# Sliding softmax mix and ELU MLP on one core: TensorE's products over halves of 64 rows, two chunks side by side

## Chip, cores and metric

One core of a Trainium2 chip runs the whole kernel. The time is the device time of one launch in microseconds; lower is better. Three runs of the kernel before gave 1204.01, 1204.09 and 1205.1 us.

## What is computed

`x` is 4 x 4096 tokens of 192 numbers, `weight_gen` has 8 heads x 7 taps for each token. Everything is float32.

```python
w = softmax(weight_gen, axis=-1)                    # with 1e-9 in the divisor
mix[b, s] = sum over k in 0..6 of w[b, s, h, k] * x_pad[b, s + k, h]   # 7 taps, 24 columns a head
h = mix @ w_in                                      # 16384 x 192 times 192 x 2048
g = where(h > 0, h, exp(min(h, 0)) - 1)             # ELU
out = g @ w_out                                     # 16384 x 2048 times 2048 x 192
```

## The kernel before

The 16384 tokens are 32 blocks of 512 (N), four tiles of 128 tokens each. The 2048 hidden columns are 16 chunks of 128. Numbers of float32 that TensorE multiplies are split in two parts that it takes at one pass each, `hi` (rounded by ScalarE's copy) and `lo` (the rest, a subtraction); of a product the parts hi hi, lo hi and hi lo are summed.

- **First product** (`first_product`, L859): for one chunk, a PSUM slot of 128 x 512 is filled by five matmuls of 512 columns. Three contract the first 128 of the 192 rows of the mix. Two contract the other 64 rows; the halves of the 128 rows that the array has there hold those 64 rows twice, as `hi` and as `lo`. Four slots go round. PE writes the slot three chunks (LAG) ahead of the chunk whose second product it does.
- **ELU**: ScalarE takes the exponential of the slot (L649) into `em`, subtracts 1 (L655), VectorE writes max(slot, min(em, 0)) into the slot (L808), ScalarE copies it rounded to `g_hi` (L662), VectorE subtracts for `g_lo` (L814).
- **Second product** (`second_product`): for each of four tiles a matmul with `g_hi` as weights against 384 columns of `wout`, which holds hi and lo side by side (L870), and one with `g_lo` against 192 (L874), into one accumulator bank a tile. In chunks 0 and 15 the two alternate tile by tile. At the end of a block ScalarE copies half of each bank to `cross` (L638) and VectorE adds the other half (L790); this runs in chunk 1 of the next block.
- **The mix**: GpSimd multiplies by the taps (L436) and adds them up (L444, L452, L453, L464, L465), VectorE transposes (L784), SyncE's queue writes to DRAM and reads back turned, ScalarE rounds (L632), GpSimd makes the low parts (L470, L473). The softmax of the block after next is shared by VectorE, GpSimd and ScalarE in steps at fixed chunks of the block.

The order on each engine is that of the code; semaphores tie the engines together.

## Time and profile before

| | |
|---|---|
| median of 3 runs | 1204.09 us |
| the profiled execution, its own time | 1204.23 us |
| its span, first to last instruction | 1202.4 us |
| granted TensorE clock | 0.998 of full speed |
| PE busy | 1183.3 us, 98% |
| weight loads (PEld) busy | 1071.6 us, 89% |
| ScalarE busy | 957.5 us, 80% |
| VectorE busy | 767.7 us, 64% |
| GpSimd busy | 779.2 us, 65% |

PE is the row of matmuls, PEld that of the loads of their weights, which overlap. Busy time is the union of what the profile shows as running. A matmul's end is modelled and reaches past the start of the next, so the start to start time of two matmuls tells more than the duration of one.

### The profile page before, as it was taken

To read this page: it belongs to the slowest core of one execution; us is meant where nothing else is said; L and a number is where in the kernel's file an instruction comes from. 1 tells how busy PE (TensorE), PEld (TensorE's weight loads), DVE (VectorE), ACT (ScalarE), POOL (GpSimd) and SP (SyncE) were. 2 spreads that over 40 slices of the span, in tenths; PEclk is the share of its full clock that TensorE was granted. 3 is DMA by queue.
4 is the path that set the end of the run, shared out by engine and by line. 5 is a ranking of instruction groups with operands and counts; after the bars stand their busy time and mean duration, and the time that the engine had idled before them with its cause. 6 is when DMAs were issued, how large, how long until landed. Compare 5 with 4: busy or idle time off the path is not lost.

```text
span 1202.4 us, 19288 instructions
## 1 busy us (share of the span) xinstructions
PE 1183.3 (98%) x6683; PEld 1071.6 (89%) x6683; DVE 767.7 (64%) x1309; ACT 957.5 (80%) x1786; POOL 779.2 (65%) x359
## 2 busy tenths in 40 slices
PE   5999999999999999999999999999999999999998
PEld 4899999999999999999999999999999999999997
DVE  6666666666656666666666566666666665666655
ACT  5888787887887887878878878878788788788786
POOL 7966785556865567765568655678555686555700
PEclk9999999999999999999999999999999999999999
DMA  7122221222111222112221112221122211221000
GB/s 236 34 81 81 65 67 31 80 81 80 52 51 58 80 80 64 66 31 80 81 80 52 51 58 80 80 64 67 31 80 80 81 51 42 67 80 44 27 31 14
DMA packets 51919, 79.37 MB, mean 66 GB/s; under 512 B 5416, under 2 KB 34852, under 8 KB 51872
## 3 DMA queue, kind: packets, MB, share of 16 engines
q1 hardware_dynamic: 51872, 78.90, 21.5%
q14 instruction: 37, 0.30, 0.1%
q8 instruction: 10, 0.16, 0.1%
HBM read 54.50 MB, written 24.38 MB: 66 GB/s over the span
## 4 chain that ended last, share of the span: by engine, by line
PE 96%; POOL 3%; DMA 0%; issue 0%; DVE 0%; SPq 0%; ACT 0%; DVEq 0%; POOLq 0%
PE slot L859 49%; PE acc L870 29%; PE acc L874 17%; POOL prod L436 1%; POOL prod L444 1%; DMA xwin<-in_x_dram 0%; POOL wout L481 0%; POOL prod L452 0%; POOL prod L453 0%; POOL win_lo L481 0%; POOL win_rest_lo L481 0%; POOL first_mixed L464 0%; POOL first_rest L465 0%; DVE outs L790 0%; PE slot L846 0%
## 5 line engine op out<-in xcount | busy, mean ns | idle before, releaser
L808 DVE SCALAR_TENSOR_TENSOR slot<-em,slot 128x512 f32<-128x512 f32 x512 | 356.3, 696 | 411.6 <-ACT em L655 406.2
L870 PE MATMUL acc<-wout,g_hi 128*128 128x384 f32 x2048 | 461.8, 338 | 0.5 <-DVE g_lo L814 0.5
L649 ACT ACTIVATE em<-slot 128x512 f32<-128x512 f32 x512 | 305.2, 596 | 187.9 <-PE slot L859 187.8
L870 PEld LDWEIGHTS acc<-wout,g_hi 128*128 128x128 f32 x2048 | 372.7, 188 | 43.0 <-issue 1.2
L814 DVE TENSOR_TENSOR g_lo<-slot,g_hi 128x512 fp32r<-128x512 f32 x511 | 349.4, 684 | 0.1
L655 ACT ACTIVATE em<-em 128x512 f32<-128x512 f32 x512 | 323.5, 632 | 16.3
L874 PE MATMUL acc<-wout,g_lo 128*128 128x192 f32 x2048 | 326.0, 266 | 0.0
L874 PEld LDWEIGHTS acc<-wout,g_lo 128*128 128x128 f32 x2048 | 311.2, 190 | 2.4
L436 POOL TENSOR_TENSOR prod<-xwin,probs 128x5376 f32<-128x5376 f32 (+1 forms) x33 | 306.6, 9294 | 6.4 <-POOL xt L473 5.2
L662 ACT ACTIVATE g_hi<-slot 128x512 fp32r<-128x512 f32 x511 | 297.1, 582 | 0.1
L859 PE MATMUL slot<-xt,win_hi 128*128 128x512 f32 (+1 forms) x515 | 215.0, 418 | 1.5 <-ACT xt L582 1.5
L859 PE MATMUL slot<-xt,win_rest_hi 128*128 128x512 f32 (+1 forms) x515 | 204.1, 397 | 0.1
L859 PE MATMUL slot<-xt_lo,win_hi 128*128 128x512 f32 (+1 forms) x515 | 202.5, 394 | 0.2 <-DVE xt_lo L759 0.2
L859 PE MATMUL slot<-xt,win_rest_lo 128*128 128x512 f32 (+1 forms) x515 | 200.3, 390 | 0.0
L859 PE MATMUL slot<-xt,win_lo 128*128 128x512 f32 (+1 forms) x515 | 199.9, 389 | 0.0
L444 POOL TENSOR_TENSOR prod<-prod 128x2304 f32<-128x2304 f32 (+1 forms) x32 | 163.4, 5106 | 2.4
L424 POOL TENSOR_TENSOR wsum<-wsum,eps 128x32 f32<-128x32 f32 x30 | 7.6, 253 | 227.4 <-DVE wsum L553 227.4
L859 PEld LDWEIGHTS slot<-xt_lo,win_hi 128*128 128x128 f32 x515 | 96.8, 188 | 22.7 <-DVE xt_lo L759 0.4
L859 PEld LDWEIGHTS slot<-xt,win_rest_lo 128*128 128x128 f32 x515 | 97.3, 189 | 22.0
L859 PEld LDWEIGHTS slot<-xt,win_rest_hi 128*128 128x128 f32 x515 | 97.1, 189 | 20.7 <-DVE xt L765 0.3
L859 PEld LDWEIGHTS slot<-xt,win_hi 128*128 128x128 f32 x515 | 99.1, 193 | 2.2 <-ACT xt L582 2.2
L859 PEld LDWEIGHTS slot<-xt,win_lo 128*128 128x128 f32 x515 | 99.3, 193 | 0.0
(70 smaller groups left out, 535.0 us busy)
## 6 DMA issues: line engine op xcount, KB each, us to landing
xwin<-in_x_dram SPq DMA_DIRECT2D x29, 960.0 KB, 5.1
out_dram<-outs SPq DMA_DIRECT2D x32, 384.0 KB, 2.6
turned_dram<-turned SPq DMA_DIRECT2D x120, 96.0 KB, 2.0
x_main<-turned_dram SPq DMA_DIRECT2D x30, 256.0 KB, 2.9
x_rest<-turned_dram SPq DMA_DIRECT2D x60, 128.0 KB, 3.0
wg<-in_weight_gen_dram SPq DMA_DIRECT2D x32, 112.0 KB, 2.5
xwin<-in_x_dram SPq DMA_DIRECT2D x2, 768.0 KB, 4.4
wout_raw<-in_moe_w_out_dram SPq DMA_DIRECT2D x4, 384.0 KB, 8.9
```

Of the source, the lines that this page charges most:

```text
L424: nc.gpsimd.tensor_tensor(wsum[:], wsum[:], eps[:], ALU.add).then_inc(s_psoft, 1)
L436: done = nc.gpsimd.tensor_tensor(prod_of(first, end), taps_of(q, first, end), weights_of(q, first, end), ALU.mult)
L444: nc.gpsimd.tensor_tensor(prod[:, 0:half, first_tile * d_model:], prod[:, 0:half, first_tile * d_model:], prod[:, half:2 * half, first_til ...
L649: nc.scalar.activation(em[:, i % 2, :], slot[s][:], ACT.Exp).then_inc(s_exp, 1)
L655: nc.scalar.activation(em[:, i % 2, :], em[:, i % 2, :], ACT.Copy, bias=-1.0).then_inc(s_em, 1)
L662: nc.scalar.activation(g_hi[:, f % GBUFS, :], slot[slot_of(b, pos - 1)][:], ACT.Copy).then_inc(s_ghi, 1)
L808: nc.vector.scalar_tensor_tensor(out=slot[s][:], in0=em[:, i % 2, :], scalar=0.0, in1=slot[s][:], op0=ALU.min, op1=ALU.max).then_inc(s_g, 1)
L814: nc.vector.tensor_tensor(g_lo[:, f % GBUFS, :], slot[slot_of(b, pos - 1)][:], g_hi[:, f % GBUFS, :].bitcast(F32), ALU.subtract).then_inc( ...
L859: return pe.matmul(slot[s][:, tokens], w, v, start=(k == 0), stop=(k == PASSES - 1))
L870: pe.matmul(acc[j][:, 0:2 * d_model], g_hi[:, f % GBUFS, chunk(j)], wout[:, f, :], start=(f == 0), stop=False)
L874: return pe.matmul(acc[j][:, d_model:2 * d_model], g_lo[:, f % GBUFS, chunk(j)], wout[:, f, 0:d_model], start=False, stop=(f == CHUNKS - 1))
```

## The change

- The 192 rows are cut in three pieces of 64. The lower half of the array's rows (0 to 63) works for chunk `2m`, the upper half (64 to 127) for chunk `2m+1`. The mix stands twice in `xt`, once in each half. The weights of even chunks lie in partitions 0 to 63, those of odd ones in 64 to 127. A pair of chunks takes 3 parts x 3 pieces x 2 halves, 18 matmuls of 64 rows and 512 columns, into two slots (`half_products`, L873 of the kernel after).
- The second product of a pair (`second_products`, L900) is done in 64-row halves as well: 16 matmuls of 384 columns with `g_hi`, then 16 of 192 with `g_lo`, in steps of four. In a step the lower half's matmul writes tile j's bank and the upper half's that of tile j+2. Each step waits on `s_row` until the step before the last is complete. The last pair of a block alternates hi and lo by step.
- PE fills the slots of pair m+1 ahead of the second product of pair m.
- In pairs 4 to 7 of a block (`low_first`) VectorE writes min(slot, 0) to `em` (L796), ScalarE takes only the exponential for the odd chunk, and VectorE's L801 subtracts 1 and takes the maximum. `cross` is gone: VectorE sums the two halves of a bank by a reduction (L789), between its two ELU steps and its two subtractions of pair 0.
- The softmax is begun three blocks ahead, the turned mix comes back as three pieces by two reads, ScalarE rounds three pieces (L635), GpSimd makes three low parts (L489), and the final sum of the mix is one instruction. The weights are split by ScalarE and VectorE alone, and w_in is loaded by six transfers a part.

```diff
+        def low_first(m):
+            return m >= PAIRS // 2
...
-            return (6, 11) if b.first else (5, 10)
+            return (4, (0, 3)) if b.first else (3, (0, 3)) if not b.has_old and b.pair == 0 else (2, (1, 2))
...
+        def softmaxes(b):
+            if not b.has_previous:
+                return {("max", 0): 2, ("exp", 1): 2, ("sum", 1): 2, ("rec", 3): 2,
+                        ("max", 5): 3, ("exp", 7): 3, ("sum", 7): 3}
+            late = 6 if b.has_old else 7
+            at = {("rec", 0): 2, ("max", 4): 3, ("exp", late): 3, ("sum", late): 3}
+            return {k: n for k, n in at.items() if number(b) + n < BLOCKS}
...
+                for m in range(PAIRS):
+                    one, two = 2 * m, 2 * m + 1
+                    exponential(b, one)
+                    if low_first(m):
+                        exponential_of_low(b, two)
+                        less_one(b, one)
+                        high(b, two)
+                        high(b, one)
                     else:
+                        less_one(b, one)
+                        exponential(b, two)
+                        less_one(b, two)
+                        high(b, one)
+                        high(b, two)
+                    if b.first and m in SPLIT_AT:
+                        hi_half(*SPLIT_AT[m])
+                    if ("exp", m) in softmax:
+                        softmax_exp(ahead(b, softmax["exp", m]))
+                    if b.has_next and m == at + 2:
+                        high_parts(b, range(pieces[0] or PIECES))
+                    if b.has_next and m == at + 3 and pieces[0]:
+                        high_parts(b, range(pieces[0], PIECES))
...
+                for j, t in enumerate(DONE):
+                    dve.wait_ge(s_row, b.count(STEPS, STEPS - TILES + 1 + j - n_before * STEPS))
+                    nc.vector.tensor_reduce(outs[:, parity, t, :],
+                                            acc[t][:, 0:2 * d_model].rearrange("p (k d) -> p d k", k=2), AX.X,
...
+            def below(b, f):
+                dve.wait_ge(s_filled, b.count(CHUNKS, f + 1))
+                nc.vector.tensor_scalar_min(em[:, 1, :], slot[slot_of(f)], 0.0).then_inc(s_low, 1)
+            def elu_of_low(b, f):
+                dve.wait_ge(s_exp, b.count(CHUNKS, f + 1))
+                nc.vector.scalar_tensor_tensor(out=slot[slot_of(f)], in0=em[:, 1, :], scalar=-1.0,
+                                               in1=slot[slot_of(f)], op0=ALU.add, op1=ALU.max).then_inc(s_g, 1)
+            def elu(b, f):
+                dve.wait_ge(s_em, ems(b, f // 2) + f % 2 + 1)
+                nc.vector.scalar_tensor_tensor(out=slot[slot_of(f)], in0=em[:, f % 2, :], scalar=0.0,
+                                               in1=slot[slot_of(f)], op0=ALU.min, op1=ALU.max).then_inc(s_g, 1)
...
+                for m in range(PAIRS):
+                    one, two = 2 * m, 2 * m + 1
+                    softmax_step("rec", m)
+                    if m == turn_at(b)[0] and b.has_next:
+                        turn(b)
+                    if low_first(m):
+                        below(b, two)
+                        elu_of_low(b, two)
+                        elu(b, one)
+                        low(b, two)
+                        low(b, one)
+                    else:
+                        elu(b, one)
+                        elu(b, two)
+                        if m == 0 and b.has_previous:
+                            dve.wait_ge(s_stored[1 - q], b.per_parity(16, 16 * q))
+                            outputs(b, 1, 1 - q)
+                        low(b, one)
+                        low(b, two)
+                    if b.first and m in SPLIT_AT:
+                        low_half(*SPLIT_AT[m])
+                    softmax_step("max", m)
+                    softmax_step("sum", m)
...
-            def one_pass(parity, f, s, k, tokens=slice(0, N)):
-                cols = chunk(f)
-                w, v = ((win_hi[:, cols], xt[:, parity, 0, tokens]), (win_lo[:, cols], xt[:, parity, 0, tokens]),
-                        (win_hi[:, cols], xt_lo[:, parity, tokens]), (win_rest_hi[:, cols], xt[:, parity, 1, tokens]),
-                        (win_rest_lo[:, cols], xt[:, parity, 1, tokens]))[k]
-                return pe.matmul(slot[s][:, tokens], w, v, start=(k == 0), stop=(k == PASSES - 1))
-            def first_product(parity, f, s):
-                for k in range(PASSES):
-                    last = one_pass(parity, f, s, k)
-                last.then_inc(s_filled, 1)
...
+            def half_products(parity, m, passes, tokens=slice(0, N)):
+                cols = chunk(m)
+                for n in passes:
+                    k = n % PIECES
+                    w, v = ((win_hi, xt), (win_lo, xt), (win_hi, xt_lo))[n // PIECES]
+                    for h, rows in enumerate(HALVES):
+                        last = pe.matmul(slot[slot_of(2 * m + h)][:, tokens], w[rows, k, cols],
+                                         v[rows, parity, k, tokens], start=(n == 0), stop=(n == PASSES - 1))
+                        if n == PASSES - 1 and tokens.stop == N:
+                            last.then_inc(s_filled, 1)
+            def second_products(b, m):
+                one, two = 2 * m, 2 * m + 1
+                hi = (g_hi, slice(0, 2 * d_model))
+                lo = (g_lo, slice(d_model, 2 * d_model))
+                highs, lows_ = ((one, hi), (two, hi)), ((one, lo), (two, lo))
+                if m == PAIRS - 1:
+                    steps = [(j, highs + lows_) for j in range(TILES)]
                 else:
-                    pe.wait_ge(s_ghi, b.count(CHUNKS, f + 1))
-                    for j in range(TILES):
-                        hi(j)
-                    pe.wait_ge(s_split, b.count(CHUNKS, f + 1))
-                    for j in range(TILES):
-                        last = lo(j)
-                    last.then_inc(s_used, 1)
+                    steps = [(j, part) for part in (highs, lows_) for j in range(TILES)]
+                pe.wait_ge(s_ghi, b.count(CHUNKS, two + 1))
+                for step, (j, products) in enumerate(steps):
+                    if m == 0 and step < 2:
+                        ge(pe, s_out, b.count(TILES, 2 * step + 2 - TILES))
+                    ge(pe, s_row, b.count(STEPS, 4 * TILES * m + 2 * step - 2))
+                    for n, (f, (g, cols)) in enumerate(products):
+                        if j == 0 and f == one and g is g_lo:
+                            pe.wait_ge(s_split, b.count(CHUNKS, two + 1))
+                        for h, rows in enumerate(HALVES):
+                            t = (j + 2 * h) % TILES
+                            last = pe.matmul(acc[t][:, cols], g[rows, f % GBUFS, chunk(t)],
+                                             wout[rows, f, 0:cols.stop - cols.start],
+                                             start=(f == 0 and g is g_hi and step < 2),
+                                             stop=(f == CHUNKS - 1 and g is g_lo and j >= 2))
+                            if n == len(products) - 1:
+                                last.then_inc(s_row, 1)
...
+                for m in range(PAIRS):
+                    n = m + 1
+                    if n < PAIRS:
+                        if not (b.first and n < 2):
+                            ge(pe, s_split, b.count(CHUNKS, 2 * (n - 1)))
+                            if b.first and n % 2 == 0:
+                                pe.wait_ge(s_wlo, SPLITS.index(("in", n // 2)) + 1)
+                            half_products(q, n, range(PASSES))
                     elif b.has_next:
-                        i = f + LAG - CHUNKS
-                        if i == 0:
-                            if b.has_previous:
-                                pe.wait_ge(s_xtlo, b.count(2))
-                            else:
-                                pe.wait_ge(s_xlo, 2 * XPARTS * X_STEPS)
-                        slot_free(len(steps) + i)
-                        first_product(1 - q, i, i % SLOTS)
-                    if not b.has_previous and f in (p.start for p in WOUT_PARTS):
-                        part = f // (CHUNKS // 4)
-                        if ("out", part) in LO_ORDER:
-                            pe.wait_ge(s_wlo, LO_ORDER.index(("out", part)) + 1)
-                        else:
-                            pe.wait_ge(s_plo, PLO_ORDER.index(("out", part)) + 1)
-                    second_product(b, f)
+                        pe.wait_ge(s_xtlo, b.count(PIECES, PIECES))
+                        pe.wait_ge(s_split, b.count(CHUNKS, CHUNKS - 2))
+                        half_products(1 - q, 0, range(PASSES))
+                    if b.first and m % 2 == 0:
+                        pe.wait_ge(s_wlo, SPLITS.index(("out", m // 2)) + 1)
+                    second_products(b, m)
```

TensorE in the middle of a block. Before, from the last matmul of a first product to the next one (a name is written tile, then `<-` and what is read):

```order
L859 MATMUL slot<-xt,win_rest_hi 128x512
L859 MATMUL slot<-xt,win_rest_lo 128x512
L870 MATMUL acc<-wout,g_hi 128x384 [waits s_ghi]
L870 MATMUL acc<-wout,g_hi 128x384 x3
L874 MATMUL acc<-wout,g_lo 128x192 [waits s_split]
L874 MATMUL acc<-wout,g_lo 128x192 x3
L859 MATMUL slot<-xt,win_hi 128x512 [waits s_split]
```

After, one pair of chunks: the rest of its first products and the first two steps of the second products:

```order
L873 MATMUL slot<-xt,win_hi 128x512 x5
L873 MATMUL slot<-xt,win_lo 128x512 x6
L873 MATMUL slot<-xt_lo,win_hi 128x512 x6
L900 MATMUL acc<-wout,g_hi 128x384 [waits s_row,s_ghi]
L900 MATMUL acc<-wout,g_hi 128x384 x3
L900 MATMUL acc<-wout,g_hi 128x384 [waits s_row]
L900 MATMUL acc<-wout,g_hi 128x384 x3
```

A chunk's 5 + 4 + 4 matmuls have become a pair's 18 + 16 + 16, and a wait on `s_row` stands ahead of each four matmuls of a second product; two more such steps with `g_hi` and four with `g_lo` follow.

VectorE at the start of a block. Before, around the four sums of the block before:

```order
L814 TENSOR_TENSOR g_lo<-slot,g_hi 128x512 [waits s_ghi]
L790 TENSOR_TENSOR outs<-acc,cross 128x192 [waits s_cross,s_stored1]
L790 TENSOR_TENSOR outs<-acc,cross 128x192 [waits s_cross] x3
L808 SCALAR_TENSOR_TENSOR slot<-em,slot 128x512 [waits s_em]
L814 TENSOR_TENSOR g_lo<-slot,g_hi 128x512 [waits s_ghi]
```

After, from the last steps of the softmax ahead of pair 0 to pair 1:

```order
L562 TENSOR_REDUCE wsum<-probs 128x32 [waits s_esoft]
L566 RECIPROCAL wrec<-wsum 128x32 [waits s_psoft]
L807 SCALAR_TENSOR_TENSOR slot<-em,slot 128x512 [waits s_em] x2
L789 TENSOR_REDUCE outs<-acc 128x192 [waits s_row,s_stored0]
L789 TENSOR_REDUCE outs<-acc 128x192 [waits s_row] x3
L813 TENSOR_TENSOR g_lo<-slot,g_hi 128x512 [waits s_ghi] x2
L807 SCALAR_TENSOR_TENSOR slot<-em,slot 128x512 [waits s_em] x2
L813 TENSOR_TENSOR g_lo<-slot,g_hi 128x512 [waits s_ghi] x2
```

The four sums now stand between the ELU steps (L807) and the subtractions (L813) of pair 0, on which PE's `g_lo` steps wait.

## Rows read from the trace of the kernel before

**Rows 1.** The page: busy time by engine, and the chain that ended last.

```profile
PE 1183.3 (98%) x6683; PEld 1071.6 (89%) x6683; DVE 767.7 (64%) x1309; ACT 957.5 (80%) x1786; POOL 779.2 (65%) x359
...
PE slot L859 49%; PE acc L870 29%; PE acc L874 17%; POOL prod L436 1%; POOL prod L444 1%; DMA xwin<-in_x_dram 0%; POOL wout L481 0%; POOL prod L452 0%; POOL prod L453 0%; POOL win_lo L481 0%; POOL win_rest_lo L481 0%; POOL first_mixed L464 0%; POOL first_rest L465 0%; DVE outs L790 0%; PE slot L846 0%
```

**Rows 2.** The waits: who waited for whom, us in total, times, longest.

```profile
DVE slot L808 <- ACT em L655: 406.2, 452, 2.0
...
ACT em L649 <- PE slot L859: 187.8, 377, 1.9
```

**Rows 3.** Timeline, one chunk and a third: start us, us, engine, line, operation, tiles.

```profile
601.54 0.60 ACT L649 ACTIVATE em<-slot 128x512 f32<-128x512 f32 x1 [0.54 <-PE slot L859]
...
602.17 0.63 ACT L655 ACTIVATE em<-em 128x512 f32<-128x512 f32 x1
...
602.46 0.42 PE L859 MATMUL slot<-xt,win_hi 128*128 128x512 f32 x1
...
602.71 0.58 ACT L662 ACTIVATE g_hi<-slot 128x512 fp32r<-128x512 f32 x1
602.72 0.39 PE L859 MATMUL slot<-xt,win_lo 128*128 128x512 f32 x1
...
602.84 0.69 DVE L808 SCALAR_TENSOR_TENSOR slot<-em,slot 128x512 f32<-128x512 f32 x1 [1.00 <-ACT em L655]
602.95 0.39 PE L859 MATMUL slot<-xt_lo,win_hi 128*128 128x512 f32 x1
...
603.41 0.39 PE L859 MATMUL slot<-xt,win_rest_lo 128*128 128x512 f32 x1
...
603.44 0.68 DVE L814 TENSOR_TENSOR g_lo<-slot,g_hi 128x512 fp32r<-128x512 f32 x1
603.64 0.86 PE L870 MATMUL acc<-wout,g_hi 128*128 128x384 f32 x4
603.84 0.60 ACT L649 ACTIVATE em<-slot 128x512 f32<-128x512 f32 x1 [0.55 <-PE slot L859]
...
604.34 0.58 PE L874 MATMUL acc<-wout,g_lo 128*128 128x192 f32 x4
...
604.76 0.42 PE L859 MATMUL slot<-xt,win_hi 128*128 128x512 f32 x1
```

**Rows 4.** Groups by line: busy us, mean ns of one, idle before and releaser.

```profile
L870 PE MATMUL acc<-wout,g_hi 128*128 128x384 f32 x2048 | 461.8, 338 | 0.5 <-DVE g_lo L814 0.5
...
L874 PE MATMUL acc<-wout,g_lo 128*128 128x192 f32 x2048 | 326.0, 266 | 0.0
...
L790 DVE TENSOR_TENSOR outs<-acc,cross 128x192 f32<-128x192 f32 x128 | 37.1, 351 | 13.7 <-ACT cross L638 12.6 <-ACT cross L682 1.1
...
L632 ACT ACTIVATE xt<-x_main 128x512 fp32r<-128x512 f32 x30 | 18.7, 624 | 0.0
...
L549 DVE TENSOR_REDUCE wmax<-wg 128x32 f32<-128x224 f32 x30 | 11.3, 377 | 0.0
```

**Rows 5.** Timeline, the last chunk: a weight load that waited, and those behind it.

```profile
1197.47 0.19 PEld L870 LDWEIGHTS acc<-wout,g_hi 128*128 128x128 f32 x1 [0.18 <-DVE g_lo L836]
1197.48 0.44 PE L870 MATMUL acc<-wout,g_hi 128*128 128x384 f32 x1
...
1197.76 0.25 PE L874 MATMUL acc<-wout,g_lo 128*128 128x192 f32 x1
...
1197.85 0.36 PE L870 MATMUL acc<-wout,g_hi 128*128 128x384 f32 x1
...
1198.04 0.25 PE L874 MATMUL acc<-wout,g_lo 128*128 128x192 f32 x1
```

**Rows 6.** Timeline of the start: w_in's transfers, and the split that waits for them.

```profile
3.06 1.18 SPq L323 DMA_DIRECT2D win_rest_raw<-in_moe_w_in_dram  x2
...
9.50 0.63 ACT L597 ACTIVATE win_hi<-win_raw 128x512 fp32r<-128x512 f32 x1 [5.48 <-DMA win_rest_raw<-in_moe_w_in_dram]
```

517 lines of the change are left out of this document (197 added, 320 removed).

## Prediction

> **What bounds the kernel now.** I read the page first. PE is busy 98% of the span, and the chain that ended last is PE through and through: 49% in the first products and 29% + 17% in the second ones [rows 1]. Next the waits: ScalarE waited 187.8 us in all for PE's slots, and VectorE 406.2 us for ScalarE [rows 2]. The helpers wait for PE and PE for nobody, so only what shortens PE's own stream counts. Last the timeline of one chunk, from start to start: the first product from 602.46 to 603.64 is 1.18 us, the four matmuls of 384 columns up to 604.34 are 0.70, the four of 192 up to 604.76 are 0.42, together 2.30 us, and 4.60 for two chunks [rows 3]. Per matmul that is 0.23 for 512 columns (0.26 for the first of the five), 0.174 for 384 and 0.105 for 192. The granted clock is 0.998 of full speed, that is the 2.4 GHz level, where a column a tick would make 0.213, 0.160 and 0.080 (the step from 384 to 512 columns, 0.056, is near the 0.053 of that). What is left for the swap of weights is 0.014 to 0.017, and more, 0.025, at 192 columns.
>
> **TensorE's stream.** I call a matmul of the lower half and the one of the upper half behind it a couple. If the two halves of a couple run side by side, it costs what one matmul of its width costs now. The first products of a pair are then 9 couples, 0.26 + 8 x 0.23 = 2.10 us, where two chunks took 2 x 1.18 = 2.36. The second products are 8 couples at 0.174 = 1.39 and 8 at 0.105 = 0.84, as long as now. The pair takes 4.33 us in place of 4.60. That is the upper end of this case: 256 pairs x 0.27 = 69 us less. The lower end lets the swap of one half's weights hide under the other half's columns: 9 x 0.213 + 8 x 0.160 + 8 x 0.09 = 3.92 us (0.09 is what a matmul of 192 columns takes between two of 384, from 1197.76 to 1197.85 [rows 5]), 0.68 x 256 = 174 us less. No row shows a 64-row matmul. The nearest rows are today's, and each half still swaps between two of its own matmuls, so I stay near the upper end, a third of the way down: 4.19 us, 0.41 x 256 = **-105 us**.
>
> A pair has 50 weight loads where it had 26. The Trainium skill ("TensorE: Matmul & The Clock Gate", LDWEIGHTS) says that a load's time goes by its columns and not by its rows, 128 columns at 1.2 GHz, so a 64-row load would cost as much as a full one. The trace agrees as far as it goes, since 0.105 us is what the narrowest matmuls need. The Trainium skill's "TensorEngine Tiling (Array Packing)" (Key Properties) says that different tiles can load and multiply in parallel; no run here shows that yet. By the second rule the sum stands; with loads that cost this much one behind the other it would be near the first rival's.
>
> **The row waits.** Each step of four matmuls waits until the step before the last is complete. For 384 columns: the last matmul of that step shows 0.338 us [rows 4], and a semaphore takes some 0.04 (PE's last matmul ends at 603.41 + 0.39 = 603.80, ScalarE starts at 603.84 [rows 3]). From its start that is 0.38, and the step that waits is due 0.174 + 2 x 0.174 = 0.52 after it. No loss. For 192 columns: 0.266 + 0.04 = 0.31 against 0.105 + 0.21 = 0.315; it arrives in time, but the weights cannot be loaded ahead. What that costs is in the last chunk: the load at 1197.47 waited for its semaphore, and the next matmul started 0.28 after its own matmul's start, against 1198.04 - 1197.85 = 0.19 for the same two undisturbed [rows 5], so 0.09. Two chains of steps interleave, so at most about 0.1 a pair, at least nothing. I take 0.05 x 256 = **+13 us**.
>
> **The helpers, pair by pair.** Let e be the end of a pair's last first-product matmul. In pairs 0 to 3, with the start to start times of [rows 3]: ScalarE's exponential at e + 0.04, minus one at 0.67, the second exponential at 1.21, its minus one at 1.84, done at 2.47; VectorE at 2.51, done at 3.20; ScalarE's `g_hi` at 3.24, done at 3.82, seen at 3.86, and with a weight load that waited, 3.95. PE is there 4.19 - 0.39 + 0.23 = 4.03 after e. The cover is 0.08 us, which is thin. Under 4.11 us a pair these four pairs would be bound by ScalarE and VectorE. In pairs 4 to 7 the chain is exponential to 0.73, VectorE's minimum beside it (not in this trace; the nearest row is its 0.69 on the same slot), exponential to 1.40, VectorE 1.41 to 2.7 for both chunks, `g_hi` of the second to be rounded done at 3.3, 3.4 with the hop; 0.6 us of cover. One minus-one of 0.63 is gone from ScalarE there; three roundings of 0.62 a block in place of two [rows 4] lie in that cover. GpSimd's and the softmax's work was moved by blocks, not by the microsecond, and GpSimd is at 65% [rows 1]; I cost it at nothing. If that cover is gone, PE waits for the turned mix at the end of a block.
>
> **The start of a block.** Here is the one wait that I see for sure. VectorE has its second ELU step of pair 0 at e + 2.51 and can go on at 3.11 (a step of 0.60). Then come four reductions of 384 numbers. None is in the trace: one of 224 numbers takes 0.377 [rows 4], one more number about 1 ns (512 numbers 0.684, 192 numbers 0.351), so 0.54 each, started every 0.46. They end at 5.03. PE's first step of pair 0 needs two of them and is about in time; its second is due at 4.03 + 0.35 = 4.38, needs all four, and starts at 5.03 + 0.04 + 0.09 = 5.16: 0.78 lost. Behind the reductions the two subtractions end at 4.95 + 0.60 + 0.68 = 6.23, and PE, at 5.16 + 3 x 0.35 = 6.19, needs them at 6.36 with hop and load: 0.17 more. Together 0.95 x 31 blocks = **+29 us**. The bounds are 0 (the adds of today, 0.351 each, cost PE nothing, but there PE had three chunks in hand) and 1.5 us a block if the strided reduction runs at 0.68.
>
> **Start and end.** w_in comes in six transfers a part where three were issued, 1.18 us for two of them, and ScalarE's first split waits 5.48 us for the data [rows 6]: +2 us. In the first block ScalarE and VectorE also split the weights that GpSimd did: +1. At the end the last pair has no first products ahead of it: its `g_hi` comes 3.95 us after e, PE has only 2.2 us of pair 6: +2. Sum **+5 us**, 2 to 10.
>
> **Sum.** From the profiled execution's own 1204.2 us (span 1202.4; the median is 0.1 less): 1204.2 - 105 + 13 + 29 + 5 = **1146 us**.
>
> **The rivals.**
> *Loads or issue queue up* (slower). If the two halves' loads, or the instructions, go one behind the other at the 0.105 us that a load and a matmul need at least today [rows 3], each couple of the second product costs 0.21 and the pair 2.10 + 16 x 0.21 = 5.46 us; +220, with PE so slow that the waits vanish: 1429 us. It decides from 0.145 us a couple. For it: no row shows two in less. Against it: that 0.105 is measured with all 128 rows in one load, and the two halves need not share it. The Trainium skill ("TensorE: Matmul & The Clock Gate", Back-to-back issue gap) has 81 ns for a load and a 128-column matmul in a stream; by an estimate from that page, 0.162 a couple of 192 columns, the time would be some 1250 us. No run here shows it.
> *Row waits cost a blocked load each* (slower). Eight a pair at 0.085 are 0.68 us: 1133 + 174 = 1307 us. It decides from three in eight. Against it: the sum above leaves 0.14 us of room at 384 columns.
> *The helpers bind.* The chain of pairs 0 to 3 is 0.25 us longer than reckoned: (0.25 - 0.08) x 128 = 22 and a little more at block starts: 1175 us, still faster.
> *The halves do not run side by side.* Then the change does not do what it says: 18 x 0.23 + 16 x 0.174 + 16 x 0.105 = 8.6 us a pair, 2230 us.
>
> **How the numbers follow.** Forecast 0.50 (own range 1080 to 1170), helpers bind 0.20 (1165 to 1200), loads or issue 0.13, row waits 0.11, not side by side 0.03, and 0.03 that gain and waits cancel. Faster 0.70, within 0.2% (which is about what a measurement here can tell) 0.03, slower 0.27. The range 1080 to 1240 holds the first two, the cancelling and the mild part of the next two, about 0.8.
>
> **What the profile after would show.** Right: the matmuls of a couple start within some 10 ns of each other, couples of 512 columns 0.21 to 0.23 apart, of 192 columns 0.08 to 0.11; PE waits once a block for VectorE's reductions, near 1 us; ScalarE waits for PE less than 187.8 us in all. Wrong: starts of a couple 0.1 us or more apart (loads or issue), or as far apart as a whole matmul (not side by side), gaps ahead of every fourth matmul (row waits), or PE waiting for `g_hi` in pairs 0 to 3 (helpers). A reduction of over 0.6 us, or a clock that PE's new gaps let fall from 1.0, would make the number wrong though the mechanism is right.

## The result, and the profile after

| | before | after |
|---|---|---|
| median | 1204.05 us (4 runs) | 1246.21 us (4 runs, 1245.63 to 1246.66) |
| span of the profiled execution | 1202.4 us | 1244.9 us |
| granted TensorE clock, mean | 0.998 | 0.99 |

The ratio is 1.0348, with a 95% interval of 1.033 to 1.0366. The changed kernel is 3.5% slower, where the forecast was 1146 us with a range up to 1240.

The page of the kernel after; the first row answers to the first of [rows 1], the second and third are the chain that ended last:

```profile
PE 1200.8 (96%) x12848; PEld 1026.3 (82%) x12848; DVE 922.7 (74%) x1431; ACT 903.0 (73%) x1549; POOL 802.3 (64%) x355
...
PE 81%; DVE 7%; ACT 5%; issue 5%; POOL 2%; DMA 0%; DVEq 0%; SPq 0%; POOLq 0%
PE acc L900 44%; PE slot L873 37%; DVE outs L789 5%; ACT em L642 3%; ACT em L652 2%; POOL prod L453 1%; DMA xwin<-in_x_dram 0%; DVE slot L807 0%; DVE win_lo L760 0%; POOL xt_lo L489 0%; DVE wout L760 0%; POOL prod L470 0%; POOL prod L469 0%; DVE acc L730 0%; PE slot L861 0%
```

PE is still the bound, but no longer alone: the chain goes through VectorE, ScalarE and GpSimd for 14% of the span, the largest part of it, 5%, in L789, the four reductions of a block. The waits of the kernel after answer to [rows 2]:

```profile
ACT em L642 <- PE slot L873: 217.9, 249, 3.1
DVE slot L807 <- ACT em L652: 173.0, 186, 3.7
...
ACT em L647 <- DVE em L796: 31.5, 126, 10.4
...
PE acc L900 <- issue: 11.3, 2, 9.2
...
PE acc L900 <- DVE outs L789: 8.5, 31, 0.3
```

ScalarE waits for PE more than before (217.9 us where it was 187.8), not less as I had written. Two rows are new: PE waits 31 times for the reductions, and one of ScalarE's waits for VectorE's minimum lasted 10.4 us.

The groups that answer to [rows 4]:

```profile
L900 PE MATMUL acc<-wout,g_hi 64*128 64x384 f32 x4096 | 434.5, 341 | 25.3 <-issue 11.3 <-DVE outs L789 8.5 <-ACT g_hi L658 5.6
...
L900 PE MATMUL acc<-wout,g_lo 64*128 64x192 f32 x4096 | 334.1, 288 | 0.1
...
L789 DVE TENSOR_REDUCE outs<-acc 128x192 f32<-128x384 f32 x128 | 62.3, 548 | 2.6 <-PE acc L900 2.6
```

**One pair of chunks.** TensorE's timeline of the kernel after, the last pair of a block, whose second products alternate hi and lo by step:

```profile
600.38 0.88 PE L873 MATMUL slot<-xt,win_hi 64*128 64x512 f32 x6
601.10 0.86 PE L873 MATMUL slot<-xt,win_lo 64*128 64x512 f32 x6
601.79 0.85 PE L873 MATMUL slot<-xt_lo,win_hi 64*128 64x512 f32 x6
602.48 0.51 PE L900 MATMUL acc<-wout,g_hi 64*128 64x384 f32 x4
602.82 0.36 PE L900 MATMUL acc<-wout,g_lo 64*128 64x192 f32 x4
...
604.74 0.65 PE L873 MATMUL slot<-xt,win_hi 64*128 64x512 f32 x4
```

Six matmuls of 512 columns take 0.69 us (601.10 to 601.79), so a couple takes 0.23. The halves do run side by side. The pair is 604.74 - 600.38 = 4.36 us, beside the 4.33 of my upper end. The same timeline where all `g_hi` steps stand ahead of the `g_lo` ones, as in pairs 0 to 6:

```profile
612.17 1.58 PE L900 MATMUL acc<-wout,g_hi 64*128 64x384 f32 x16
...
613.58 1.27 PE L900 MATMUL acc<-wout,g_lo 64*128 64x192 f32 x16
...
614.69 0.88 PE L873 MATMUL slot<-xt,win_hi 64*128 64x512 f32 x6
```

The 16 matmuls with `g_hi` take 1.41 us (I had reckoned 1.39), but the 16 with `g_lo` take 1.11 where I had 0.84. Such a pair takes 4.61 us, the 4.60 of two chunks before: all that the halves gain is lost again in the `g_lo` steps. Narrow windows on these 16 matmuls give the start of each step; here are the second and the fourth:

```profile
613.83 0.36 PE L900 MATMUL acc<-wout,g_lo 64*128 64x192 f32 x2
...
614.39 0.36 PE L900 MATMUL acc<-wout,g_lo 64*128 64x192 f32 x2
```

The eight couples of `g_lo` start at 613.58 and 613.68 (first step), 613.83 and 614.02 (second), 614.13 and 614.25 (third), 614.39 and 614.58 (fourth), and the next first product at 614.69. Where nothing waits they stand 0.10 to 0.12 apart. The second and the fourth step start 0.15 and 0.14 behind the couple ahead of them, and in both the second couple comes 0.19 behind the first. Each of these two steps loses some 0.12 us; the first and the third lose nothing.

**One block.** Read in this way from start to start of the first products, the eight pairs of each block from the third on take 4.61, 4.35, 5.33, and then five times 4.61; from 563.02 to 600.38 that is 37.36 us, where a block before took 36.75 (1102.40 / 30). The 5.33 is the stretch with pair 0's second products:

```profile
605.72 1.95 DVE L789 TENSOR_REDUCE outs<-acc 128x192 f32<-128x384 f32 x4
...
606.87 0.61 PE L900 MATMUL acc<-wout,g_hi 64*128 64x384 f32 x4
...
607.59 1.28 DVE L813 TENSOR_TENSOR g_lo<-slot,g_hi 128x512 fp32r<-128x512 f32 x2
607.60 9.71 POOL L453 TENSOR_TENSOR prod<-xwin,probs 128x5376 f32<-128x5376 f32 x1 [0.16 <-POOL probs L448]
...
607.80 1.32 PE L900 MATMUL acc<-wout,g_hi 64*128 64x384 f32 x12 [0.32 <-DVE outs L789]
```

The reductions end at 607.67 (605.72 + 1.95), PE's second step starts at 607.80, and the stretch is 0.72 us longer than the others. That wait is the one that was forecast (0.95).

**The first 100 us.** Busy time and granted clock by stretch, before and after:

```profile
0.00:50.00 50.00, 34.42 (x176) 29.62 (x177) 32.43 (x57) 36.22 (x68) 42.90 (x31) 0.97 0.52 162
50.00:100.00 50.00, 50.00 (x287) 45.37 (x286) 32.77 (x60) 39.41 (x79) 38.27 (x15) 1.00 0.16 49
```

```profile
0.00:50.00 50.00, 31.06 (x284) 27.05 (x284) 41.48 (x48) 25.96 (x43) 41.08 (x24) 0.93 0.50 152
50.00:100.00 50.00, 38.07 (x374) 33.10 (x372) 35.05 (x49) 29.20 (x51) 29.45 (x12) 0.86 0.23 62
```

The columns are the stretch, its length, busy us (and instructions) of PE, PEld, VectorE, ScalarE and GpSimd, the granted clock, the DMA share and GB/s. PE is busy 12 us less in the second stretch than before, and its clock is 0.86 there. Four rows of the timeline say why:

```profile
44.45 9.71 POOL L453 TENSOR_TENSOR prod<-xwin,probs 128x5376 f32<-128x5376 f32 x1 [0.27 <-POOL probs L448]
...
44.80 10.17 DVE L760 TENSOR_TENSOR win_lo<-win_raw,win_hi 128x768 fp32r<-128x768 f32 x1
...
59.22 2.93 PE L900 MATMUL acc<-wout,g_hi 64*128 64x384 f32 x16 [9.20 <-issue]
59.88 0.96 DVE L760 TENSOR_TENSOR wout<-wout_raw,wout 128x768 fp32r<-128x768 f32 x1
```

A subtraction for the weights' low parts takes VectorE 0.96 us at 59.88 and 10.17 us at 44.80. It starts just behind a product of GpSimd's and ends at 54.97, 0.81 us after that product's end at 54.16. VectorE's ELU steps are queued behind it, ScalarE waits 10.4 us for the minimum, and PE stands for 9.20 us. After that its 16 `g_hi` matmuls need 2.70 us from start to start (59.22 to 61.92), 1.9 times the 1.41 of later; the granted clock from 59.2 to 61.9 is 0.50, which is the 1.2 GHz level and not the 2.4.

**The sum.** PE runs ahead with its first products, so a block is counted here up to the start of its last first product (that of pair 7, or of chunk 15 before). "Start" is the start of the very first one, and "rest" is what follows the last one:

| | start | blocks 0, 1 | 30 blocks | rest | span |
|---|---|---|---|---|---|
| before | 13.54 | 76.76 | 1102.40 | 9.7 | 1202.4 |
| after | 14.86 | 95.13 | 1120.99 | 13.92 | 1244.9 |
| difference | +1.3 | +18.4 | +18.6 | +4.2 | +42.5 |

And for a later block: eight pairs at 4.36 would be 34.88, 1.87 less than before. The `g_lo` steps of seven pairs add 1.76 and the reductions 0.72. So a gain of 1.87 stands against a loss of 2.48: +0.61, which is 18.3 over thirty blocks. In the rest, the last pair's first `g_hi` step starts at 1236.74, and PE had stood 0.98 us for it; its second products then take 4.2 us, at a granted clock of 0.65, where the same pair takes 2.26 in the steady blocks.

### The profile page after: what moved, and what is told of

Read it like the earlier page. It is cut to its first block, busy times and chain, and to the rows that moved or that the text cites. A ratio compares the mean times of both kernels' runs of the same rounds, so it can differ in the third digit from the quotient of the medians.

```text
span 1244.9 us, 33016 instructions
## 1 busy us (share of the span) xinstructions
PE 1200.8 (96%) x12848; PEld 1026.3 (82%) x12848; DVE 922.7 (74%) x1431; ACT 903.0 (73%) x1549; POOL 802.3 (64%) x355
## 4 chain that ended last, share of the span: by engine, by line
PE 81%; DVE 7%; ACT 5%; issue 5%; POOL 2%; DMA 0%; DVEq 0%; SPq 0%; POOLq 0%
PE acc L900 44%; PE slot L873 37%; DVE outs L789 5%; ACT em L642 3%; ACT em L652 2%; POOL prod L453 1%; DMA xwin<-in_x_dram 0%; DVE slot L807 0%; DVE win_lo L760 0%; POOL xt_lo L489 0%; DVE wout L760 0%; POOL prod L470 0%; POOL prod L469 0%; DVE acc L730 0%; PE slot L861 0%
## 5 line engine op out<-in xcount | busy, mean ns | idle before, releaser
L900 PE MATMUL acc<-wout,g_hi 64*128 64x384 f32 x4096 | 434.5, 341 | 25.3 <-issue 11.3
L900 PEld LDWEIGHTS acc<-wout,g_hi 64*128 64x128 f32 x4096 | 337.4, 186 | 86.3 <-issue 23.6
L807 DVE SCALAR_TENSOR_TENSOR slot<-em,slot 128x512 f32<-128x512 f32 x384 | 266.4, 695 | 173.4 <-ACT em L652 173.0
L642 ACT ACTIVATE em<-slot 128x512 f32<-128x512 f32 x384 | 227.5, 592 | 217.9 <-PE slot L873 217.9
L489 POOL TENSOR_TENSOR xt_lo<-x_raw,xt 128x512 fp32r<-128x512 f32 x93 | 118.5, 1290 | 371.2 <-ACT xt L635 371.2
L813 DVE TENSOR_TENSOR g_lo<-slot,g_hi 128x512 fp32r<-128x512 f32 x512 | 346.5, 689 | 5.5
L900 PE MATMUL acc<-wout,g_lo 64*128 64x192 f32 x4096 | 334.1, 288 | 0.1
L900 PEld LDWEIGHTS acc<-wout,g_lo 64*128 64x128 f32 x4096 | 298.9, 188 | 34.6 <-PE acc L900 6.8
L873 PE MATMUL slot<-xt,win_hi 64*128 64x512 f32 (+1 forms) x1548 | 226.6, 398 | 2.0 <-ACT xt L592 1.3
L873 PE MATMUL slot<-xt,win_lo 64*128 64x512 f32 (+1 forms) x1548 | 221.0, 390 | 0.0
L873 PE MATMUL slot<-xt_lo,win_hi 64*128 64x512 f32 (+1 forms) x1548 | 218.0, 387 | 0.0
L873 PEld LDWEIGHTS slot<-xt,win_lo 64*128 64x128 f32 x1548 | 145.7, 186 | 33.9
L873 PEld LDWEIGHTS slot<-xt_lo,win_hi 64*128 64x128 f32 x1548 | 145.6, 185 | 32.7
L801 DVE SCALAR_TENSOR_TENSOR slot<-em,slot 128x512 f32<-128x512 f32 x128 | 89.1, 696 | 89.4 <-ACT em L647 89.4
L873 PEld LDWEIGHTS slot<-xt,win_hi 64*128 64x128 f32 x1548 | 127.8, 189 | 14.1 <-issue 1.0
L796 DVE TENSOR_SCALAR em<-slot 128x512 f32<-128x512 f32 x128 | 88.5, 691 | 37.4 <-PE slot L873 36.0
L789 DVE TENSOR_REDUCE outs<-acc 128x192 f32<-128x384 f32 x128 | 62.3, 548 | 2.6 <-PE acc L900 2.6
```

Of the source, the lines that this page charges most:

```text
L489: nc.gpsimd.tensor_tensor(by_tile(xt_lo[:, parity, k, :]), by_quad(x_raw[:, k, :]), by_tile(xt[:, parity, k, :].bitcast(F32)), ALU.subtrac ...
L642: nc.scalar.activation(em[:, f % 2, :], slot[slot_of(f)], ACT.Exp).then_inc(s_exp, 1)
L789: nc.vector.tensor_reduce(outs[:, parity, t, :], acc[t][:, 0:2 * d_model].rearrange("p (k d) -> p d k", k=2), AX.X, ALU.add).then_inc(s_ou ...
L801: nc.vector.scalar_tensor_tensor(out=slot[slot_of(f)], in0=em[:, 1, :], scalar=-1.0, in1=slot[slot_of(f)], op0=ALU.add, op1=ALU.max).then_ ...
L807: nc.vector.scalar_tensor_tensor(out=slot[slot_of(f)], in0=em[:, f % 2, :], scalar=0.0, in1=slot[slot_of(f)], op0=ALU.min, op1=ALU.max).th ...
L813: nc.vector.tensor_tensor(g_lo[:, f % GBUFS, :], slot[slot_of(f)], g_hi[:, f % GBUFS, :].bitcast(F32), ALU.subtract).then_inc(s_split, 1)
```

## The experiments

My theory after the result had three parts: the row waits cost about 0.25 us a pair, the reductions 0.72 us a block, and VectorE's blocked splits, with the fallen clock, most of the 18 us of the first two blocks. The rivals were that the `g_lo` steps are slow by their loads or by their banks, that the start is slow for other reasons, and that the losses are not independent.

### Row waits or banks

In pairs 0 to 6 each half of the array keeps two banks of its own, so the two halves never write the same bank and the waits can go without a race. (The banks then hold other sums.) The control has the same banks and keeps the waits.

```diff
-                    ge(pe, s_row, b.count(STEPS, 4 * TILES * m + 2 * step - 2))
+                    if m == PAIRS - 1:
+                        ge(pe, s_row, b.count(STEPS, 4 * TILES * m + 2 * step - 2))
...
-                            t = (j + 2 * h) % TILES
+                            t = (j + 2 * h) % TILES if m == PAIRS - 1 else j % 2 + 2 * h
```

> A measuring kernel: in pairs 0 to 6 the lower half of the array adds into banks 0 and 1 alone and the upper half into banks 2 and 3 alone, so the two never meet in a bank and the waits on s_row ahead of the steps are left out there. The sums land in the wrong tiles, so the output is not the reference's; the instructions, their widths and their number stay. Theory A (the row waits make the narrow steps late): the 16 matmuls of 192 columns take 0.84 us in place of 1.11, a pair 4.33 to 4.36 in place of 4.61, and 7 pairs x 32 blocks x 0.26 = 58 us go: about 1188 us. Theory B (0.07 us is the least for a load and a matmul of 64 rows, whatever waits): the pair stays at 4.61 and the time at 1246 us.

> The same banks as the kernel without the row waits, but with the waits left in: the sums land in the wrong tiles here too. It tells the banks' own effect from that of the waits. Both theories: 4.61 us a pair, 1246 us. If it is faster than that, the choice of banks and not the wait sets the pace.

Measured, one run each: 1194.82 us without the waits, 1242.34 with them, 47.5 us apart; the banks alone make 3.9 us (1246.21 to 1242.34). The timeline of the first one:

```profile
600.78 1.57 PE L901 MATMUL acc<-wout,g_hi 64*128 64x384 f32 x16
602.19 1.03 PE L901 MATMUL acc<-wout,g_lo 64*128 64x192 f32 x16
603.06 0.88 PE L873 MATMUL slot<-xt,win_hi 64*128 64x512 f32 x6
```

The `g_lo` steps take 0.87 us, near the 0.84 of my sum, and the pair 4.37. The waits are the cause and the banks are not. One reason that it is 47.5 and not 7 x 32 x 0.25 = 56 is pair 0, where PE waits for the reductions as well: it comes down only from 5.33 to 5.15, so the two losses of that pair overlap.

### Keep row waits, but give them room

Matmuls with `g_hi` and `g_lo` alternate in pairs 1 to 7, as they did in pair 7 alone. Four of `g_hi` and four of `g_lo` make one step now, so a pair has four row waits in place of eight, and each looks back over a whole step of eight matmuls.

```diff
+    MIXED = 1
...
-                if m == PAIRS - 1:
+                if m >= MIXED:
                     steps = [(j, highs + lows_) for j in range(TILES)]
```

> Undoes one part of the change for pairs 1 to 6: their second product alternates g_hi and g_lo tile by tile, as only the last pair of a block does in the changed kernel (there a pair takes 4.36 us against 4.61). Both theories: pairs 4 to 7 take 4.36 us. In pairs 1 to 3 g_lo is needed earlier than it is there: it comes 4.67 us after the first product's end, which makes a pair 4.48 us. A block is then 37.36 - 3 x 0.25 - 3 x 0.13 = 36.2 us, 31 blocks 36 us less: about 1210 us. Rival: the wait for g_lo eats the gain in pairs 1 to 3 in full, then 0.75 a block is left and 1223 us.

Measured: 1202.39 us, ratio to the kernel before 0.9982 (0.9972 to 0.9991). TensorE's timeline:

```profile
600.89 0.51 PE L905 MATMUL acc<-wout,g_hi 64*128 64x384 f32 x4
601.24 0.37 PE L905 MATMUL acc<-wout,g_lo 64*128 64x192 f32 x4
601.45 0.53 PE L905 MATMUL acc<-wout,g_hi 64*128 64x384 f32 x4
```

Four hi and four lo matmuls together take 0.56 us (600.89 to 601.45) and the pairs 4.36, but for pair 0's 5.33 and one a block at 4.51; I had expected three at 4.48, so it came out 8 us better. 43.8 us come back from the order of the matmuls, with the banks and the sums as they were. The edit changes two things together, the number of waits and the room of each, and no run separates them.

### Is the rest of the stream bound by loads?

`g_lo` meets 96 columns of `wout` in place of 192, once in the kernel without row waits and once in the kernel before. Half of the lo products is left out.

> A measuring kernel on top of the one with own banks and no row waits: the g_lo matmuls of 64 rows have 96 columns in place of 192 (the output is not the reference's: sums in the wrong tiles and half of the g_lo term left out). There 16 of 192 columns took 0.87 us, 0.109 a couple. If the loads of weights set that pace, each half loading its own, it stays at 0.107 a couple and the kernel at 1195 us. If the columns did, it falls to 0.06 a couple, a pair to 3.98 us, and 256 x 0.38 = 97 us go, as far as the helpers allow (they need 4.11 us in pairs 0 to 3): about 1110 to 1130 us.

> The kernel before with 96 columns in place of 192 in its g_lo matmuls of 128 rows (half of the g_lo term is left out, so the output is not the reference's). If a load of 128 rows takes the 0.105 us that these matmuls show, nothing changes: 1204 us. If the columns or a fixed cost beside them set it, four of them take 0.26 in place of 0.42 us and 512 x 0.16 = 82 us go: 1122 us. It tells whether g_lo's matmuls were bound by their loads before the change, and so what the 64-row halves could win or lose there.

Measured, one run each: 1197.93 us beside the 1194.82 with 192 columns, and 1211.17 us beside 1204. Half the columns give next to nothing back. In the changed kernel's variant the thirty later blocks take 1069.7 us in place of 1072.4, and the longer time comes from the first two, where the granted clock from 50 to 100 us is 0.76 and not 0.90; in the variant of the kernel before the same blocks take 1109.2 in place of 1102.4. The timelines, first of the changed kernel's variant, then of the variant of the kernel before:

```profile
601.79 0.99 PE L901 MATMUL acc<-wout,g_lo 64*128 64x96 f32 x16
602.61 0.93 PE L873 MATMUL slot<-xt,win_hi 64*128 64x512 f32 x6
```

```profile
600.70 0.54 PE L874 MATMUL acc<-wout,g_lo 128*128 128x96 f32 x4
601.08 0.46 PE L859 MATMUL slot<-xt,win_hi 128*128 128x512 f32 x1
601.38 0.40 PE L859 MATMUL slot<-xt,win_lo 128*128 128x512 f32 x1
```

Eight couples in 0.82 us are 0.103 a couple; four full matmuls in 0.38 are 0.095 each. The two differ only because the first of a row of narrow ones is followed after 0.05: from the second on they start 0.11 apart in both, and in the kernel without row waits the couples of 192 columns do too. So the columns do not set the pace of the narrow matmuls. A couple has two loads of 64 rows, which start together in the trace (both at 604.65 in the changed kernel), and takes the time of one load and matmul of 128 rows: the loads of the two halves also go side by side. That it is the load that sets the 0.11, and not another cost that every matmul has, is likely but not shown. What is saved there is given back in the next first product (0.30 in place of 0.26, and 0.77, from 602.61 to 603.38, in place of 0.72 for six).

### The reductions at the start of a block

The first of the four reductions goes between VectorE's two ELU steps of pair 0, where VectorE waits for ScalarE.

```diff
                         elu(b, one)
+                        if m == 0 and b.has_previous:
+                            dve.wait_ge(s_stored[1 - q], b.per_parity(16, 16 * q))
+                            outputs(b, 1, 1 - q, (0,))
                         elu(b, two)
                         if m == 0 and b.has_previous:
-                            outputs(b, 1, 1 - q)
+                            outputs(b, 1, 1 - q, (1, 2, 3))
```

> VectorE's four reductions at a block's start: the first one now stands between its two ELU steps of pair 0, where it waits for ScalarE anyway, and three stand behind. Theory (PE's 0.72 us a block is the wait for the fourth reduction and for the subtractions behind it): both come 0.46 us sooner, the wait shrinks to about 0.3, 31 x 0.4 = 12 us go: 1234 us. Rival: the first bank isn't complete in time, the second ELU step is late for it, g_hi too, and nothing is won or a little lost: 1246 to 1252 us.

Measured: 1231.10 us, ratio 1.0224 (1.0207 to 1.0241), 15.1 us under the changed kernel. VectorE's timeline:

```profile
596.47 0.70 DVE L809 SCALAR_TENSOR_TENSOR slot<-em,slot 128x512 f32<-128x512 f32 x1 [1.51 <-ACT em L652]
...
597.08 0.55 DVE L791 TENSOR_REDUCE outs<-acc 128x192 f32<-128x384 f32 x1
597.63 0.70 DVE L809 SCALAR_TENSOR_TENSOR slot<-em,slot 128x512 f32<-128x512 f32 x1
598.23 1.48 DVE L791 TENSOR_REDUCE outs<-acc 128x192 f32<-128x384 f32 x3
```

The last three reductions take 1.48 us in place of 1.95 for four. The stretch is 4.87 in place of 5.33 and the block 36.84 in place of 37.36: 0.5 x 31 = 15.

### VectorE's blocked splits

GpSimd's products for the mix are issued in quarters, so that VectorE waits for one of some 2.7 us and not for 9.7. First for all blocks:

```diff
-                products(q, 0, TILES)
+                for t in range(TILES):
+                    products(q, t, t + 1, last=t == TILES - 1)
```

> GpSimd's large multiplication (9.7 us) is issued as four of a tile each, in every block. Theory: VectorE's splits of the weights in block 0 (L760, both inputs in SBUF) stand still while a GpSimd instruction that reads SBUF runs, and one of them lasts 10.17 us for that reason, beside 3.44 and 4.01; with quarters none lasts over 3.5 us, PE's gap of 9.2 us before pair 4 of block 0 shrinks by 7 us, and the time is about 1238 us. Rival (the splits are slow by themselves, or VectorE waits out all four parts one after the other): the split still lasts 10 us and the time stays at 1246 us or rises by what four smaller instructions cost GpSimd, which has the room.

Measured: 1237.33 us (1234.16 to 1249.42), ratio 1.0263 (1.0239 to 1.0287). One split still lasts 5.83 us, longer than the 3.5 that I had named as the most: it stands beside the pair sum of 5.16 us, which this edit leaves whole. Then for blocks 1 and 2 alone, with the pair sum of block 1 in quarters too:

> The changed kernel, with GpSimd's products for blocks 1 and 2 issued in quarters (and the pair sum of block 1 too), all later blocks as they were. Theory (VectorE's weight splits read SBUF twice and stand still as long as one GpSimd instruction runs beside them, PE then waits and its clock falls): as in the kernel with quarters everywhere, no split of the weights takes over about 6 us, blocks 0 and 1 come to some 89 us in place of 95, and without the extra instructions of the later blocks the time is 1236 to 1240 us. Rival (the gain of the kernel with quarters everywhere came from later blocks): blocks 2 to 31 stay at 37.3 us and the time stays at 1246 us.

Measured: 1240.57 us (1233.73 to 1252.3), ratio 1.0281 (1.0251 to 1.0311) without the longest. VectorE's timeline of the second one, three of its five splits:

```profile
26.10 1.43 DVE L770 TENSOR_TENSOR wout<-wout_raw,wout 128x768 fp32r<-128x768 f32 x1
...
40.95 1.17 DVE L770 TENSOR_TENSOR win_lo<-win_raw,win_hi 128x768 fp32r<-128x768 f32 x1
48.85 1.47 DVE L770 TENSOR_TENSOR wout<-wout_raw,wout 128x768 fp32r<-128x768 f32 x1
```

The splits that took 3.44, 4.01, 2.11, 10.17 and 0.96 us take 1.43, 2.20, 1.24, 1.17 and 1.47, and the first two blocks 82.5 us in place of 95.1. So the splits are blocked as long as one instruction of GpSimd's lasts, and that is shown. The 12.6 us from there would make 1233.6, and the lowest times of the two kernels are 1234.16 and 1233.73. The medians are higher because both kernels scatter, so that a median near the one expected proves little. Their profiled executions are the longest of each, and have two and three pairs that take 8.7 to 9.0 us in place of 4.35 (with the pair behind them, 5 to 6.7 us lost each time). The profile puts PE's pause down to VectorE's `g_lo`, but the one that PE's code asks for there was done long before: 327.87 for a pause from 330.6 to 335.05. The loop instructions of PE (L109) tell more. In the window 329 to 336 of the second kernel:

```profile
L109 PEldq COMPARE_BRANCH  x1: 5077/5077/5077, 329.8 to 329.8; - x1
```

The branch that closes PE's loop over the blocks lasts 5.08 us there and 0.21 as a rule. All five pauses are such branches, of 4.73 to 5.08 us, and the changed kernel's 14 take 0.24 at most. So PE stands at the turn of its own loop; no other engine is shown that holds it. What the branch waits for is open. The row of DMA queue 8, which carries instructions, has 47 packets in this execution and 38 in the other, and 20 in the changed kernel's:

```profile
q8 instruction: 47, 0.77, 0.3%
```

That would fit a branch that waits for the instructions behind it, but no run shows it. The quarters alone don't bring it about: the kernel with all three repairs below has them too, has 19 packets, and its four times lie within 1.6 us.

### VectorE's minimum of PSUM

Pairs 4 to 7 do their ELU steps as pairs 0 to 3 do; the minimum (L796) and L801 are gone and ScalarE subtracts the 1.

```diff
         def low_first(m):
-            return m >= PAIRS // 2
+            return False
```

> Undoes VectorE's minimum alone: all pairs go as pairs 0 to 3, with two exponentials from the slot and two times minus one on ScalarE. Theory (at 4.61 us a pair ScalarE has 0.45 us to spare on its way to g_hi): only pair 5, with two roundings of the mix, runs over, by about 0.5 us: 30 x 0.5 = 15 us more, 1261 us. Rival (the minimum is needed in no pair, since the helpers keep up at this pace): 1246 us. Second rival (ScalarE binds all over): over 1290 us.

Measured: 1244.11 us, ratio 1.0332 (1.0315 to 1.0349). The pairs that took 4.61 stay at 4.60. The theory that the minimum carries these pairs fell and its rival held: at 4.6 us a pair ScalarE has the time for the step that VectorE took over.

### All three repairs, and the minimum again

> The changed kernel with hi and lo steps alternating in pairs 1 to 7, and VectorE's first reduction between its two ELU steps of pair 0. Theory (row waits and the start of a block are two separate losses): they add, 44 us from the one and 15 from the other, so 1202.4 - 15 = 1187 us, block period near 35.5 us. Rival (with pairs at 4.36 us VectorE has less room, so that the first ELU steps of pair 0, now later, hold PE up): the second gain shrinks to under 5 us, 1198 us or more.

> As the kernel with alternating steps and the moved reduction, and GpSimd's products for blocks 1 and 2 in quarters. Theory: the three losses add, 1187 - 7 = about 1180 us, 2% faster than the kernel before. Rival (at the start of the launch another wait takes the place of the one removed): no less than 1185 us.

> As the kernel with all three edits, without VectorE's minimum of PSUM: pairs 4 to 7 do their ELU steps as pairs 0 to 3 do. At 4.61 us a pair the minimum made no difference. Theory: at 4.36 us the chain of ScalarE and VectorE in pairs 1 to 3, the same as it would now be in 4 to 7, keeps up (those pairs measured 4.36 with alternating steps), but pairs 4 to 7 also carry the softmax and the roundings of the mix on ScalarE, 0.63 us more a pair: up to 0.2 us lost in two or three of the eight pairs, 15 us, so 1195 us. Rival (the minimum is not needed at this pace either): the same as with it, 1180 us.

| kernel | median, us | ratio to before, 95% |
|---|---|---|
| alternating, reduction between | 1188.47 | 0.9868 (0.9851 to 0.9884) |
| the same, early quarters | 1177.68 | 0.9775 (0.9759 to 0.9792) |
| the same, without the minimum | 1190.96 | 0.9888 (0.9872 to 0.9905) |

The losses add: 1202.39 - 15.1 = 1187.3 was to be expected and 1188.47 came; the early quarters give 10.8 more (7 were expected). The kernel with all three is 2.2% faster than the one before. Its page, and its second stretch:

```profile
PE 1148.0 (98%) x12848; PEld 1027.3 (87%) x12848; DVE 905.5 (77%) x1431; ACT 897.4 (76%) x1549; POOL 806.8 (69%) x364
...
PE 93%; POOL 4%; DVE 2%; DMA 0%; ACT 0%; issue 0%; SPq 0%; DVEq 0%; POOLq 0%
```

```profile
50.00:100.00 50.00, 46.62 (x498) 42.03 (x498) 35.32 (x57) 34.91 (x61) 35.77 (x18) 0.95 0.26 70
```

The chain is 93% PE again. The second stretch has PE busy 46.62 us at a clock of 0.95, where it was 38.07 at 0.86. A block takes 35.53 us, 1.2 less than before, but the first two still take 82.9 where they took 76.8, and the rest behind the last block 13.0 where it was 9.7.

Without the minimum the kernel is 13.3 us slower and a block takes 36.02. VectorE now waits 340.1 us for ScalarE's `em` at this line (146.0 with the minimum, and 90.0 at the line that goes with it), and PE's loads wait 24.4 us for `g_lo` in place of 6.9:

```profile
DVE slot L824 <- ACT em L667: 340.1, 440, 2.2
...
PEld acc L919 <- DVE g_lo L830: 24.4, 98, 0.4
```

So the minimum is worth nothing at 4.6 us a pair and 13 us at 4.36.

## Why the prediction was wrong

The sum failed at two of its terms, TensorE's stream by 46 us and the row waits by 43. Either alone would have left a faster kernel, 1192 or 1189 us; together they make it slower. A third, start and end, by 19, carries the time past the range.

- **TensorE's stream (-105 forecast).** The halves run side by side, as forecast, and so do their loads. Of the two ends the upper one was right: 4.36 us a pair, not 4.19. No swap of weights is seen to hide under the other half's columns: a couple of 512 columns takes 0.23 and one of 192 takes 0.11, as one full matmul did. The term should have been (4.59 - 4.36) x 256 = -59, with 4.59 as an eighth of the 36.75 of a block. The third of the way toward 3.92 that I went had no row behind it.
- **The row waits (+13 forecast, "at most about 0.1 a pair").** They cost 0.25 us in a pair. Removing them gave 47.5 us and the other order 43.8. My own numbers would have come closer. I compared steps of 384 columns with each other and steps of 192 with each other, and left out the seam: the second `g_lo` step waits for the last `g_hi` step, whose matmul takes 0.338 and not 0.266. And I counted the weight load that cannot be moved ahead once a pair, where it comes with each step that is late. The trace shows two such steps, the second and the fourth with `g_lo` (which waits for the second), each some 0.12 us late: 0.03 to 0.04 at its start and 0.085 at the couple behind. The rival of row waits had the right mechanism with the wrong width: it counted eight blocked loads a pair at 0.085 and gave 1307. Two steps at 0.12 make what it would have called three loads, and three was the number from which it said that it decides.
- **The start of a block (+29 forecast).** The mechanism was right, place and engines too. The reduction takes 0.548 us, the estimate was 0.54. With e at 602.64 (601.79 + 0.85), PE's second step was forecast at e + 5.16 and starts at 607.80, which is e + 5.16. But with a pair of 4.36 and not 4.19 it was due 0.17 later than I had it, so 0.61 is lost and not 0.78; the late steps' loads add some 0.1. The last term of 0.17, the wait for `g_lo`, came to almost nothing: the first `g_lo` step is some 0.06 late (609.01), and the row waits of that pair lose less by as much. PE lost 0.72 us, so 22 us.
- **The helpers (nothing forecast).** In the changed kernel they cost nothing in the steady blocks, which the run without the minimum bears out. How true the 0.08 us of cover was is not shown, since no pair came down to 4.19. With the other order and the minimum gone, two of pairs 4 to 7 take 4.5 and 4.7 in place of 4.36, so at that pace the cover of those pairs is gone.
- **Start and end (+5 forecast).** Measured are +1.3 at the first start, +18.4 in the first two blocks and +4.2 at the end, 24 in all. I costed the splits that moved to VectorE at +1 by their length alone. They read SBUF twice, and beside GpSimd's product each lasts until that product is done: 10.17 us where it needs 0.96. The Trainium skill ("SBUF — State Buffer", Who interferes with whom) says that a VectorE instruction with two SBUF inputs contends with a GpSimd one that reads SBUF, and calls the ports that they share an exclusive lock. The trace agrees in all four blocked splits (3.44, 4.01, 2.11 and 10.17 us), each of which ends 0.8 us after the GpSimd instruction that ran when it started, and in the contrast too: VectorE's subtraction for `g_lo`, one input of which is in PSUM, takes 1.28 us for two at 607.59 beside the same 9.71 us product. I had not asked this of the edit that moved the splits. The fallen clock adds to it, here and in the last pair.
- **The sum.** With the measured terms: 1204 - 59 (stream) + 56 (row waits, 0.25 x 7 x 32) + 22 (reductions) + 24 (start and end) = 1247, and 1 of it is counted twice, since the difference of the first two blocks holds their stream and waits too. 1246 were measured. How the loss of pair 0 is shared between row waits and reductions is a choice: without row waits its stretch still lies 0.78 over the others.

The first rival (loads or issue queue up) fell: couples of 192 columns take 0.11 us, not 0.145 or more. So did the last (not side by side). With the first goes the estimate of 0.162 us a couple that I had from the Trainium skill ("TensorE: Matmul & The Clock Gate", Back-to-back issue gap), 81 ns for a load and a matmul of 128 columns in a stream. Here two matmuls of 96 columns, one for each half, with their loads take 0.103 together.

What stays open: what the loop's branch waits for in the two kernels with quarters, whether fewer row waits or more room for each gives the 43.8 us, and how much of the 6 us that the best kernel still loses in the first two blocks is the fallen clock.

## What to carry to other kernels

A semaphore wait that "arrives just in time" is not free: ask it of every step against the one that it really waits for, the seams between long and short steps too, add the weight load that it keeps from going ahead, and count how often it comes. An order with fewer and longer steps can give the loss back. When work is moved to another engine, ask for each instruction which memory its inputs are in and what long instruction can run beside it, not only how long it is. And a helper's saving is worth what PE's pace makes of it: the minimum on VectorE was worth 0 at 4.6 us a pair and 13 us at 4.36.

## What the runs showed of the hardware

- Two matmuls of 64 rows on the two halves of the array, with their weight loads, take together what one of 128 rows takes: 0.23 us for 512 columns, 0.176 for 384 (0.174 for the full one) and 0.11 for 192 and for 96.
- Below 192 columns a matmul gets no cheaper here: with 96 in place of 192 both kernels keep the 0.11 us from start to start, and neither time fell (1197.93 beside 1194.82, 1211.17 beside 1204).
- A step of four `g_lo` matmuls that waits until shortly before its turn loses some 0.12 us, 0.03 to 0.04 at its start and 0.085 at the couple behind it. All row waits together cost 47.5 us (1242.34 beside 1194.82).
- A VectorE subtraction with both inputs in SBUF stood still until GpSimd's running instruction was done, 10.17 us in place of 0.96, while those with one input in PSUM ran on at their usual 0.69 us.
- After a pause of 9.20 us TensorE's next 16 matmuls took 1.9 times as long as in the steady state, at a granted clock of 0.50.
- The branch at the turn of PE's loop took 0.21 us as a rule and 4.73 to 5.08 us in five cases of two executions.
